# Two fold blocks moved ahead of a branch and of the last batch's ranks; a weight subtraction moved behind the item table; fills split over two queues

## The reference

```python
def _moe_ref(x, w_gate, w1, w2):
    logits = x @ w_gate
    expert_idx = np.argmax(logits, axis=1)
    ...
    for e in range(E):
        mask = expert_idx == e
        h = np.maximum(x[mask] @ w1[e], 0.0)
        out[mask] = gate_w[mask, None] * (h @ w2[e])

def _moe2_ref(x, w1, w2, w3, w_out):
    h = (x @ w1) * (x @ w2) @ w3
    return h @ w_out
```

## Time and profile before

| | |
|---|---|
| median of 3 runs | 996.95 us (996.77, 996.95, 999.02) |
| profiled execution | 999.18 us, its span 997.4 us |
| mean granted clock of TensorE | 0.988 of full |
| busy: TensorE, its weight loads | 919.1 us (92%), 813.5 us (82%) |
| busy: VectorE, ScalarE, POOL | 446.1 (45%), 410.0 (41%), 398.3 us (40%) |
| chain that ended last, by engine | TensorE 70%, VectorE 14%, POOL 6%, issue 5%, ScalarE 4% |

### The profile page before, as it was taken

How to read it: one execution, slowest core, us unless ns; L and a number is a source line. 1 busy time by engine, 2 the same in 40 slices (tenths; PEclk the granted TensorE clock), 3 DMA queues, 4 the chain that set the end, 5 groups by cost and what they waited for, 6 DMA issues and landing times.

```text
span 997.4 us, 17948 instructions
## 1 busy us (share of the span) xinstructions
PE 919.1 (92%) x6799; PEld 813.5 (82%) x6799; DVE 446.1 (45%) x705; ACT 410.0 (41%) x618; POOL 398.3 (40%) x230
## 2 busy tenths in 40 slices
PE   2889989789898699999999999998999999999996
PEld 2579888788787567889999999997898989898986
DVE  4888899799785531432222222222313131313130
ACT  5879888778572322322223223221313131212121
POOL 6647755965854416647256627700010101010101
PEclk9999999999999899999999999999999999999999
DMA  9624452553282346343353444301010101000000
GB/s 240 135 54 84 81 105 59 127 104 67 72 272 100 101 163 233 116 164 104 104 167 105 124 154 155 125 25 48 0 65 0 64 1 64 1 32 1 32 1 32
DMA packets 160152, 91.82 MB, mean 92 GB/s; under 512 B 128576, under 2 KB 152896, under 8 KB 160064
## 3 DMA queue, kind: packets, MB, share of 16 engines
q1 hardware_dynamic: 147344, 67.81, 25.4%
q10 hardware_dynamic: 9648, 13.30, 4.1%
q0 software_dynamic: 3072, 9.49, 2.4%
HBM read 71.77 MB, written 18.81 MB: 91 GB/s over the span
## 4 chain that ended last, share of the span: by engine, by line
PE 70%; DVE 14%; POOL 6%; issue 5%; ACT 4%; another core or an unknown queue 1%; ACTq 0%; DVEq 0%; POOLq 0%
PE psum L1929 20%; PE psum L1888 13%; PE psum L1866 13%; PE psum L1941 10%; PE psum L425 6%; PE psum L1771 3%; DVE arena L1169 2%; DVE arena L1247 2%; PE psum L1706 1%; DVE arena L1198 1%; PE psum L1732 1%; POOL x_by_expert L715 1%; POOL arena L684 1%; DVE wfold_half L1581 1%; DVE arena L1177 1%
## 5 line engine op out<-in xcount | busy, mean ns | idle before, releaser
L1929 PE MATMUL psum<-x2t,ring 128*128 128x512 f32 x864 | 197.1, 389 | 0.0
L1929 PEld LDWEIGHTS psum<-x2t,ring 128*128 128x128 f32 x864 | 162.1, 188 | 33.4
L425 PE MATMUL psum<-arena 128*128 128x128 f32 x925 | 127.6, 279 | 31.4 <-DVE arena L1169 19.1
L818 POOL DMA_INDIRECT out_dram<-arena x24 | 23.1, 962 | 320.9 <-ACT arena L1147 317.4
L425 PEld LDWEIGHTS psum<-arena 128*128 128x128 f32 x925 | 107.5, 143 | 47.4 <-POOL arena L652 19.0
L1866 PE MATMUL psum<-ring,f_xt 128*128 x558 | 137.3, 400 | 4.4 <-DVE f_xt L1555 4.4
L1888 PE MATMUL psum<-ring,f_ht 128*128 x744 | 138.7, 341 | 2.0 <-DVE f_ht L1561 2.0
L1888 PEld LDWEIGHTS psum<-ring,f_ht 128*128 128x128 f32 x744 | 129.7, 190 | 2.4 <-issue 2.3
L1866 PEld LDWEIGHTS psum<-ring,f_xt 128*128 128x128 f32 x558 | 103.7, 190 | 26.0 <-issue 4.9
L1596 DVE TENSOR_TENSOR ab_f<-psum,a_sb 128x512 f32<-128x512 f32 x48 | 33.2, 692 | 204.6 <-ACT a_sb L1137 204.6
L1941 PE MATMUL psum<-wfold_half,ab 128*128 128x384 f32 x576 | 102.8, 336 | 0.0
(11 more groups left out here) (180 smaller groups left out, 1372.6 us busy)
## 6 DMA issues: line engine op xcount, KB each, us to landing
stage<-in_moe_w_dram SPq DMA_DIRECT2D x16, 1536.0 KB, 7.2
y_dense<-arena ACTq DMA_DIRECT2D x31, 194.0 KB, 3.1
arena<-x_by_expert ACTq DMA_DIRECT2D x28, 194.0 KB, 2.4
arena<-y_dense SPq DMA_DIRECT2D x24, 194.0 KB, 3.5
arena<-in_a_re_dram SPq DMA_DIRECT2D x24, 192.0 KB, 3.8
arena<-in_a_im_dram SPq DMA_DIRECT2D x24, 192.0 KB, 3.7
arena<-in_q_dram SPq DMA_DIRECT2D x24, 192.0 KB, 2.6
arena<-in_k_dram SPq DMA_DIRECT2D x24, 192.0 KB, 3.3
```

The lines of the kernel that those rows point to most:

```text
L425: return nc.tensor.transpose(psum[:, bank, c0:c0 + P], src, ident)
L1929: last = mm(psum[:, bank + j % 2, :], m_half[m][x][:, kc, j * P:(j + 1) * P], x2t[y][:, kc, :], start=(kc == 0 and x + y == 0), stop=(kc = ...
```

## The change

On TensorE, block 2's transposes now stand ahead of `rows_t(23)`, block 3's transposes and block 2's `fold` ahead of the last ranks, block 4's transposes and block 3's `fold` ahead of the branch. `fold_t(2)` has a new wait for the last masks of attention (`att_masked`), since it writes into the banks of the scores, and the wait for `x_done` moves with `fold(2)`. ScalarE's copies move along: `fold_cols(2)` ahead of `rows_out(23)`, `fold_cols(3)`, `fold_rows(2)` and `fold_cols(4)` ahead of its branch. In the loop behind the branch, ScalarE now does `fold_rows(i)` first and `fold_cols(i + 2)` after it. POOL's subtraction for expert 0 moves from behind the last scatter to behind `table_ready`. The last three of the eight fills are issued by ScalarE, behind `fold_cols(6)`, with a wait there for the table. Nothing is added or left out in the work.

```diff
@@ SP
-            for e in range(E):
+            for e in range(E - 3):
                 row = sp.value_load(fill_i[0:1, e:e + 1], ...)
                 sp.dma_start(xs_d[bass.ds(row, P), :], fill_row).then_inc(filled, 16)
@@ POOL
             scatter_rows(B - 1, 0, C)
-            pool.wait_ge(w_split[0], 1)
-            nc.gpsimd.tensor_tensor(w1_ring[1][:, 0], stage[0], w1_ring[0][:, 0].bitcast(fp32), ALU.subtract
-                                    ).then_inc(w_split[0], 1)
             pool.wait_ge(bad_ready, 1)
...
             pool.wait_ge(table_ready, 1)
+            pool.wait_ge(w_split[0], 1)
+            nc.gpsimd.tensor_tensor(w1_ring[1][:, 0], stage[0], w1_ring[0][:, 0].bitcast(fp32), ALU.subtract
+                                    ).then_inc(w_split[0], 1)
             pool.wait_ge(fold_done, NJ)
@@ ScalarE
+            fold_cols(EARLY, m3t_late)
             rows_out(NT - 1)
             exp_logits(B - 1)
+            fold_cols(EARLY + 1, m3t_late)
+            fold_rows(EARLY, fold_out_late)
+            fold_cols(EARLY + 2, m3t_late)
             act.wait_ge(bad_ready, 1)
...
-            fold_cols(EARLY, m3t_late)
-            for i in range(EARLY, NJ):
-                if i + 1 < NJ:
-                    fold_cols(i + 1, m3t_late)
-                if i == EARLY:
-                    act.wait_ge(y_done, K * U)
-                    act.wait_ge(kt_done, K * U)
-                    upper_first(1)
-                if i < NJ - 1:
-                    fold_rows(i, fold_out_late)
+            def fill_rows(e):
+                row = act.value_load(fill_i[0:1, e:e + 1], ...)
+                act.dma_start(xs_d[bass.ds(row, P), :], fill_row).then_inc(filled, 16)
+
+            act.wait_ge(y_done, K * U)
+            act.wait_ge(kt_done, K * U)
+            upper_first(1)
+            fold_rows(EARLY + 1, fold_out_late)
+            fold_cols(EARLY + 3, m3t_late)
+            for i in range(EARLY + 2, NJ - 1):
+                fold_rows(i, fold_out_late)
+                if i + 2 < NJ:
+                    fold_cols(i + 2, m3t_late)
+                if i == EARLY + 2:
+                    act.wait_ge(table_ready, 1)
+                    act.wait_ge(fill_ready, 1)
+                    for e in range(E - 3, E):
+                        fill_rows(e)
@@ TensorE, fold_t
+                    if i == EARLY and half == 0:
+                        pe.wait_ge(att_masked, 2 * K * U)
@@ TensorE
+            fold_t(EARLY, m3_late)
             rows_t(NT - 1)
+            fold_t(EARLY + 1, m3_late)
+            pe.wait_ge(x_done, NT)
+            fold(EARLY, m3t_late, mo_late)
             rank_rows(B - 1, rank_done, hot_done)
+            fold_t(EARLY + 2, m3_late)
+            fold(EARLY + 1, m3t_late, mo_late)
             pe.wait_ge(bad_ready, 1)
...
-            pe.wait_ge(x_done, NT)
-            fold_t(EARLY, m3_late)
-            for i in range(EARLY, NJ):
-                if i + 1 < NJ:
-                    fold_t(i + 1, m3_late)
-                    fold(i, m3t_late, mo_late)
+            for i in range(EARLY + 2, NJ - 1):
+                fold_t(i + 1, m3_late)
+                fold(i, m3t_late, mo_late)
```

More of the change, by code:

```diff
@@ L1052, in _ @@
                     nc.scalar.activation(ex, lg, ACT.Exp).then_inc(g_exp, 1)
-            fold_cols(EARLY, m3t_late)
-            for i in range(EARLY, NJ):
-                if i + 1 < NJ:
-                    fold_cols(i + 1, m3t_late)
-                if i == EARLY:
-                    act.wait_ge(y_done, K * U)
-                    act.wait_ge(kt_done, K * U)
-                    upper_first(1)
-                if i < NJ - 1:
-                    fold_rows(i, fold_out_late)
+            def fill_rows(e):
+                row = act.value_load(fill_i[0:1, e:e + 1], min_val=e * CAP, max_val=e * CAP + N)
+                act.dma_start(xs_d[bass.ds(row, P), :], fill_row).then_inc(filled, 16)
[13 more added lines that the diff above has]
+                        fill_rows(e)
             def load_rows(i):
```

## The result

The changed kernel took 985.24 us in median of 4 runs (984.74 to 986.29), the kernel before 996.86 us in 4 (994.12 to 999.02): a ratio of 0.9883, interval 0.9858 to 0.9908. In two later comparisons, of 6 runs each against 29 and 17 of the kernel before, the ratio was 0.9898 (0.9876 to 0.9921) and 0.9877 (0.9849 to 0.9904). So the gain in medians is 11.6, 10.9 and 12.2 us. Forecast were 8.7 us (988.3 us), with a range down to 986.6: the direction and the mechanism were right, the gain was larger than the range allowed.

What follows compares the result with a forecast made beforehand. TensorE's idle time and low clock behind attention were taken as the bound: 7.12 us gaps plus 2.03 us clock, 9.15 us; counted as 9.1 less 0.4, 8.7 us off 996.95 gives 988.3 us, range 986.6 to 993.6.

Steps and rivals of the forecast that it cites:

- The three gaps go: TensorE behind attention: idle gaps of 0.69, 2.97 and 3.46 us before rows_t(23), last ranks and count matmul, together 7.12 us.
- The branch is hidden: TensorE's sequencer runs ahead and takes the branch while fold(3) is in the array; costed at nothing, otherwise 3.46 us and its clock.
- The table: VectorE's item table takes 6.3 us, ready at 351.2 us; first item's rows land with 1.1 us to spare.
- 0.4 us set aside: Allowance for ScalarE's copy for which fold(4) waits and for small waits, taken off 9.1 us to give 8.7 us.
- The term for the low clock, 2.03 us: TensorE behind the gaps: 1.73 us lost on 16 transposes and 0.30 us on the count matmul at 1.2 GHz.
- From there the same distance to the end.: Everything behind the first item is shifted and not changed, including TensorE's 3.46 us stall in front of item 5.
- The bare branch: Rival: branch taken only after fold(3), so 3.46 us gap and 1.8 us clock return; gain 3.4 us, 993.5 us; chance 0.12.
- Late fetches: Rival: instructions come late, two microseconds on each branch; gain 5 to 7.5 us, 989.5 to 992 us; chance 0.2.
- A table that bounds: Same rival as late fetches: the table, delayed by 1.6 us or more, becomes the bound; chance 0.2.
- the third rival's wait of ScalarE: ScalarE waits for a far later table amid the folds, holding fills, fold_rows(5) and first rows' copy; 1000 us; chance 0.03.
- Less at the clock: Rival: shorter runs of before lost less to low clock, up to 2 us; 990.3 us; chance within the forecast's 0.65.

Runs made afterwards that it cites:

- branch_bare: Changed kernel with one more wait: TensorE may load the branch's flag only once fold(3) has left the array; 997.55 us, ratio 0.9963 to the kernel before.
- folds_only: Changed kernel with POOL's subtraction back behind the last scatter and all eight fills on SP, so only fold blocks moved; 999.39 us, ratio 1.0013 to the kernel before.
- before: The kernel before the change, first comparison; 996.86 us in median of 4 runs.
- after: The changed kernel, first comparison; 985.24 us, ratio 0.9883 to the kernel before.
- after_again: The changed kernel run once more, no edit; 987.06 us, ratio 0.9898 to the kernel before.
- after_third: The changed kernel run a third time, no edit; 988.21 us, ratio 0.9877 to the kernel before.
- sub_back: Changed kernel with POOL's weight subtraction alone back behind the last scatter; 996.03 us, ratio 0.9951 to the kernel before.
- fills_back: Changed kernel with all eight fills back on SP; 993.51 us, ratio 0.9922 to the kernel before.
- sub_only: Kernel before with only POOL's weight subtraction moved behind the table; 998.37 us, ratio 1.0000 to the kernel before.
- lower_at_2: Changed kernel with the folded weights' upper and lower part made at item 2 instead of 3; 986.65 us, ratio 0.9852 to the kernel before.
- before_warm: Kernel before with 22 and 28 spare transposes filling most of two idle stretches on TensorE; 1001.30 us, ratio 1.0013 to the kernel before.

## Why the prediction was wrong in size, and right in kind

*The three gaps go.* Right: 7.12 us of idle time are gone, none took their place.

*The branch is hidden.* Right, and shown from both sides: the row of L1835 beside the fold, and branch_bare, in which the cover is taken away. The evidence of L1851's row (the sequencer passes a whole fold in 0.2 us) carried over to a branch. The DMA view of the kernel before has, in 336 to 338 us, a single transfer, of 0.02 MB on an instruction queue, about 1 us behind the start of the branch at 335.1; the same stands about 1 us behind the start of the branch in the changed kernel (337.5 us) and in branch_bare (348.0 us). This agrees with the Trainium skill's rule that a taken branch to a target outside the fetched window waits for a DMA fetch of its page ("Runtime: NRT & Kernel Launch", instruction fetch mechanics); which fetch the transfer was, the rows do not say. Matmuls that were already queued covered it.

*The table.* Right: 6.1 us for 6.3, slack 0.6 us for 1.1. The two smaller parts are not idle beside the folds; they are what lets the folds pay, 6.5 and 3.3 us. The sum had them as a slack that stays positive, which is the same thing, and folds_only is what it would have been without.

*0.4 us set aside.* Not needed: `fold_rows(3)` ran at 341.14 us, just as the fold ended. And two small pieces were shorter when they followed without a gap (`rows_t` and ranks 0.87 and 0.60 us from start to next start, instead of 1.14 and 0.87). Together 0.9 us more than the forecast in the same stretch: 9.6 instead of 8.7. That alone, 987.3 us, would have been inside the range.

*The term for the low clock, 2.03 us.* This is the step that failed, here and in the next paragraph. It was read off one execution of the kernel before, for which it is right (7.1 of gaps, 0.5 and 2.0 of clock are its 9.6 us), and I took it as a constant. It varies between executions: the clock was low for 6.8, 10.2, 10.2 and 10.2 us in the four profiles with TensorE's old order, and the stretch was 48.2, 48.7, 49.8 and 48.9 us. Their mean of 48.9 less 38.6 is 10.3 us. Of these some 6.9 are the three gaps (7.1, 6.4, 7.3 and 6.9 us) and 0.5 the two pieces, which leaves 2.9 for the clock.

*"From there the same distance to the end."* Wrong too, and the larger part of the miss: the sum put the low clock behind the first item at no change, and it measured 1.8 us. From the first item to the dense network it was 308.5, 307.8 and 309.7 us in the three profiles of before and its like, and 306.7 to 306.9 in after, after_again, after_third, sub_back and fills_back. The stall itself is the same 3.46 us; the low clock behind it lasted 3.4, 6.8 and 6.8 us in the former and 3.4 in each of the latter, and two of the former had one more low clock at 680 to 685 us (before and sub_only), as lower_at_2 had at 666 us. This time follows the low clock alone in all the profiles with the stall: 306.7 to 306.9 us with 3.4 us of it, 307.8 to 307.9 with 6.8, and 1.6 to 1.9 us more where one more came behind 660 us. Why the former have more is open: folds_only and branch_bare, whose TensorE idles elsewhere, had 6.8 us at the stall as well, before_warm, in TensorE's old order, 3.4. It goes with an earlier low clock in the stretch in most profiles but not in all (sub_back had 6.8 and 3.4), and no run here tells a cause from chance. That the change itself brought these 1.8 us is not shown.

Stretch and items together make 10.3 + 1.8 = 12.1 us, against 11.6, 10.9 and 12.2 measured in medians. The difference is within the scatter: 29 runs of the kernel before lay between 995.5 and 1003.9 us. The clock's part is seen without any profile too. With span x (1 - mean clock) as the measure of what the low clock costs (too high, since it counts idle time too), the kernel before loses 16.2 us in mean of 29 runs and the changed one 10.9 in 6; the rest of the span has medians of 980.2 and 975.2 us. That is half of the gain at most; the profiles give 2.9 + 1.8 = 4.7 us of 12.1, where my sum gave it 2 us of 9.

*The rivals.* The bare branch was priced at 5.3 us and costs 8.8: the gap was 5.46 us for 3.46, and the clock took some 3.3 for 1.8. Late fetches: the load and the branch were 0.25 us and 0.2 us longer than before, which nothing noticed. A table that bounds did not come, but by 0.6 us; in sub_back the third rival's wait of ScalarE is seen at work. "Less at the clock" leaned the wrong way: the other executions of the kernel before lost more, not less.

*The range.* Its low end allowed one low clock less. The low clock in the stretch and behind the stall each varied by 3.4 us or more between executions, and 3.4 us at half the clock are up to 1.7 us of time, so it should have reached some 3 us further down. The three runs known then, 2.3 us apart, did not show that spread; the profiles' low clock would have, had I read it in more than one.

## What to carry to other kernels

Price an idle stretch of TensorE as its length plus the low clock behind it, and take the latter as a spread, not as one profile's number: here 7 us of gaps cost about 10 in their own stretch. Put a branch, or whatever the sequencer must do alone, right behind matmuls that are few instructions and long in the array, not behind many short ones. And before a wait goes into a queue that other work shares, as the wait for the table did on ScalarE, ask what stops if it comes late. And where a chain of small operations hides beneath the work that you move away, move its obstacles in the same step: the folds alone and the subtraction alone gave nothing, and the change without the subtraction or without the split of the fills gave less than half and some two thirds of the gain.

## What the runs showed of the hardware that was not expected

- The low clock behind the same idle stretch lasted 6.8 us in one execution and 10.2 us in three others; behind a stall of 3.46 us it lasted 3.4 or 6.8 us.
- The same taken branch on TensorE took 3.31 to 4.23 us in the fourteen profiles (3.40 in before, 3.63 in after, 4.23 in branch_bare), in all of them with a transfer on an instruction queue 1 to 1.5 us behind its start. VectorE's record of its branch is 0.07 us in the kernel before, but the engine's next instruction came 4.6 us after its last one, 2 us after the count was over. The 4.8 us in the changed kernel say nothing of the branch: there it was the count that came last.
- 28 short transposes in front of it put off the load of a branch's flag by 1.8 us, though the array was not through with them.
- A VectorE subtraction with two inputs in SBUF and POOL's one did not run beside each other here, and the row of the one that waits contains the wait: 7.60 and 6.50 us on VectorE for work of 0.39 us, 7.98 us for work of 3.35, and 9.72 us on POOL for 6.7. In most pairs the one whose row starts first went first, but not in all: in the earlier trace rows VectorE's row starts 0.65 us ahead of POOL's, and it is VectorE that waited.
